# The second MLP of an attention and two-MLP kernel in six groups of 512 tokens in place of eight of 384

## The reference

```python
for t in range(S):                       # B, H, S, D = 4, 8, 768, 48
    cur = np.einsum('bhd,bhe->bhde', u[None] * kt, vt)
    y[:, :, t] = np.einsum('bhd,bhde->bhe', rt, state + cur)
    state = wt[:, :, :, None] * state + np.einsum('bhd,bhe->bhde', kt, vt)
x = attn_out.transpose(0, 2, 1, 3).reshape(B * S, H * D)      # (3072, 384)
h = x @ w_in;  g = where(h > 0, h, exp(min(h, 0)) - 1);  x = g @ w_out
h = x @ w_in2; g = h / (1 + exp(-1.702 * h));            out = g @ w_out2
```

## Time and profile before

| | |
|---|---|
| median of 3 runs | 1113.54 us (1112.53 to 1447.67) |
| span of the profiled execution | 1110.7 us |
| what lies around the span, by the median | 2.8 us |
| TensorE busy | 1047.1 us (94%) |
| VectorE busy | 645.4 us (58%) |
| ScalarE busy | 487.4 us (44%) |
| mean granted clock of TensorE | 0.972 |

### The profile page before, as it was taken

One profiled execution on the slowest core, in us unless ns is written; L12 is line 12 of the kernel. 1 busy time (PEld: TensorE's weight loads), 2 busy tenths in 40 slices (PEclk: granted clock), 3 DMA queues, 4 the chain that ended last, 5 costly groups with the idle time before them and its releaser, 6 DMA issues. The chain is left out here.

```text
span 1110.7 us, 27196 instructions
## 1 busy us (share of the span) xinstructions
PE 1047.1 (94%) x10912; PEld 946.3 (85%) x10912; DVE 645.4 (58%) x1587; ACT 487.4 (44%) x987; POOL 71.9 (6%) x55
## 2 busy tenths in 40 slices
PE   2658999999899999999999999999999999999998
PEld 1447878888788887778887799999999999999998
DVE  7997677677567677577676544343434433343433
ACT  2444455456245446346445357633333333333332
POOL 5450000000000000000000005410000000000000
PEclk9657999999999999999999999999999999999999
DMA  6453122212212212212211313300000000000000
GB/s 168 112 131 76 42 57 56 55 45 55 57 45 55 55 45 56 56 45 55 55 45 34 134 70 93 92 1 22 1 21 0 21 22 0 21 0 22 1 23 22
DMA packets 24096, 54.56 MB, mean 49 GB/s; under 512 B 3248, under 2 KB 15792, under 8 KB 23984
## 3 DMA queue, kind: packets, MB, share of 16 engines
q1 hardware_dynamic: 22704, 46.66, 16.1%
q0 software_dynamic: 1280, 6.29, 1.9%
HBM read 39.96 MB, written 12.98 MB: 48 GB/s over the span
## 5 line engine op out<-in xcount | busy, mean ns | idle before, releaser
L1200 PE MATMUL psum<-x_hi,w_split 128*128 128x384 f32 x912 | 232.6, 336 | 0.0
L1211 PE MATMUL psum<-g_hi,w_split 128*128 128x384 f32 x912 | 232.6, 336 | 0.0
L841 PE MATMUL psum<-g_hi,w_split 128*128 128x384 f32 x624 | 172.6, 348 | 0.0
L1200 PEld LDWEIGHTS psum<-x_hi,w_split 128*128 128x128 f32 x912 | 165.0, 188 | 0.0
L1211 PEld LDWEIGHTS psum<-g_hi,w_split 128*128 128x128 f32 x912 | 164.8, 188 | 0.0
L1118 DVE TENSOR_TENSOR gate<-expo,psum 128x384 f32<-128x384 f32 x128 | 70.9, 554 | 160.8 <-ACT expo L1037 160.8
L823 PE MATMUL psum<-x_hi,w_split 128*128 128x384 f32 x624 | 161.4, 340 | 0.0
L1200 PE MATMUL psum<-x_lo,w_split 128*128 128x384 f32 x456 | 153.6, 337 | 0.0
L1211 PE MATMUL psum<-g_lo,w_split 128*128 128x384 f32 x456 | 153.2, 336 | 0.0
L1037 ACT ACTIVATE expo<-psum 128x384 f32<-128x384 f32 x128 | 63.0, 492 | 170.6 <-PE psum L1200 170.6
L1124 DVE TENSOR_TENSOR g_lo<-gate,g_hi 128x384 fp32r<-128x384 f32 x152 | 84.9, 559 | 90.0 <-ACT g_hi L1044 90.0
(11 more groups left out here) (85 smaller groups left out, 1234.8 us busy)
## 6 DMA issues: line engine op xcount, KB each, us to landing
raw<-rkwu_dram SPq DMA_DIRECT2D x32, 288.4 KB, 5.5
staging<-weights_dram POOLq DMA_DIRECT2D x16, 384.0 KB, 3.7
raw<-rkwu_dram SPq DMA_DIRECT2D x32, 144.0 KB, 4.5
v_sb<-v_tokens_dram SPq DMA_DIRECT2D x16, 288.0 KB, 2.9
y_scratch<-y_sb SPq DMA_DIRECT2D x64, 72.0 KB, 1.8
staging<-y_scratch SPq DMA_DIRECT2D x7, 576.0 KB, 4.5
out_dram<-o_sb SPq DMA_DIRECT2D x7, 576.0 KB, 3.0
x_scratch<-x_sb SPq DMA_DIRECT2D x6, 576.0 KB, 3.4
```

The costliest lines, as they stand in the source:

```text
L841: mm = pe.matmul(mlp_bank(FT + m, x), w_tile((1 - x) * FT + f, lo, (KT + m) * P), gg[:, f, :], start=at == 0, stop=at == 3 * FT - 1)
L1200: mm = pe.matmul(hidden(f), w_tile(f, lo, kt * P), xx, start=n == 0, stop=n == 3 * KT - 1)
L1211: mm = pe.matmul(acc(q, m), w_tile(f, lo, (KT + m) * P), gg, start=f == first_tile(g) and n == 0, stop=f == NF - 1 and n == 2)
```

## The change

The second MLP has WIDES = 6 groups of WIDE = 512 tokens, so each of its matmuls has 512 columns, the width of a PSUM bank. `x2` becomes one row of tokens for each third of the features, from which a group takes 512 neighbours; three DMAs bring its six groups. `PAIRS` is 3. The first MLP keeps groups of 384.

To have the room, `gate2` has one buffer in place of two, and DVE waits for the low part of the tile before it writes the next gate; the two output buffers share their memory with `scores`, `kt_sb` and `state` of the attention; and `ur` (128 x 2 x 2 x 384) becomes `uk` (128 x 2 x 384): the bonus scales k, of which there is one array, and not r, which is laid out twice (once for each of two heads).

```diff
+WIDE = 512
+WIDES = B * S // WIDE
...
-        self.scores = sb("scores", [P, U, NG, CH])
-        self.kt_sb = sb("kt_sb", [P, U, NCH * P])
-        self.state = sb("state", [P, 2, U, NCH + 1, D])
+        pile = [sb(f"pile{q}", [P, KT * WIDE]) for q in range(2)]
+        self.scores = pile[0][:].rearrange("p (u g t) -> p u g t", u=U, g=NG)
+        self.kt_sb = pile[1][:, 0:U * NCH * P].rearrange("p (u n) -> p u n", u=U)
+        self.state = pile[1][:, U * NCH * P:].rearrange("p (x u c e) -> p x u c e", x=2, u=U, c=NCH + 1)
...
-    ur = sb("ur", [P, U, 2, HALF])
+    uk = sb("uk", [P, U, HALF])
...
-                act.activation(ur[:, u], r_of(x, u), ACT.Copy, scale=u_col(x, u)).then_inc(ur_done, 1)
+                act.activation(uk[:, u, :], k_of(x, u), ACT.Copy, scale=u_col(x, u)).then_inc(uk_done, 1)
...
-            dve.tensor_scalar(out=ur[:, 1], in0=r_of(0, 1), scalar1=u_col(0, 1), scalar2=None,
-                              op0=ALU.mult).then_inc(ur_done, 1)
+            dve.tensor_scalar(out=uk[:, 1, :], in0=k_of(0, 1), scalar1=u_col(0, 1), scalar2=None,
+                              op0=ALU.mult).then_inc(uk_done, 1)
...
-                                  kk[:, o:o + 32], ur[:, u, :, o:o + 32], start=True, stop=True)
+                                  uk[:, u, o:o + 32], r[:, :, o:o + 32], start=True, stop=True)
...
-    x2 = sb("x2", [P, GROUPS, KT * N])
-    expo = sb("expo2", [P, 2, N])
-    gate = sb("gate2", [P, 2, N])
-    g_hi = sb("g_hi2", [P, 4, N], F32R)
-    g_lo = sb("g_lo2", [P, 4, N], F32R)
-    o_sb = [sb(f"o_sb{q}", [P, KT, N]) for q in range(2)]
-    x_raw = o_sb[0]
+    x2 = sb("x2", [P, KT, GROUPS * N])
+    expo = sb("expo2", [P, 2, WIDE])
+    gate = sb("gate2", [P, WIDE])
+    g_hi = sb("g_hi2", [P, 4, WIDE], F32R)
+    g_lo = sb("g_lo2", [P, 4, WIDE], F32R)
+    o_sb = [z[:].rearrange("p (k n) -> p k n", k=KT) for z in kept.pile]
+    x_raw = kept.pile[0][:, 0:KT * N].rearrange("p (k n) -> p k n", k=KT)
...
-    hidden = lambda f: psum[:, f % 2, 0:N]
-    acc = lambda q, m: psum[:, 2 + 3 * q + m, 0:N]
-    PAIRS = GROUPS // 2
+    width = lambda second: WIDE if second else N
+    hidden = lambda f, second: psum[:, f % 2, 0:width(second)]
+    acc = lambda q, m, second: psum[:, 2 + 3 * q + m, 0:width(second)]
+    PAIRS = WIDES // 2
...
-            sp.dma_start(x2[:, 0:RIDERS, :], x2_dram.rearrange("g p n -> p g n")).then_inc(x2_in, 16)
+            for k in range(KT):
+                sp.dma_start(x2[:, k, 0:RIDERS * N].rearrange("p (g n) -> p g n", g=RIDERS),
+                             x2_dram[:, :, k * N:(k + 1) * N].rearrange("g p n -> p g n")).then_inc(x2_in, 16)
...
             def chain(g, f, second):
                 j = number(g, f)
+                if not (type(j) is int and j == 0):
+                    dve.wait_ge(lo_done, j)
                 dve.wait_ge(exp_done, j + 1)
                 if second:
-                    dve.tensor_tensor(gate[:, f % 2, :], expo[:, f % 2, :], hidden(f), ALU.mult).then_inc(gate_done, 1)
+                    dve.tensor_tensor(gate[:, 0:width(second)], expo[:, f % 2, 0:width(second)], hidden(f, second), ALU.mult).then_inc(gate_done, 1)
...
             with pe.Fori(0, PAIRS - 1) as b:
                 for q in range(2):
                     group(b * 2 + q + REST, q, True, True)
-            group(REST + GROUPS - 2, 0, True, True)
-            group(REST + GROUPS - 1, 1, True, None)
+            group(REST + WIDES - 2, 0, True, True)
+            group(REST + WIDES - 1, 1, True, None)
```

More of the change, by code:

```diff
@@ L734, in near @@
                 n = i * 2 + x
-                pe.wait_ge(ur_done, n * U + (U if first else u + 1))
+                pe.wait_ge(uk_done, n * U + (U if first else u + 1))
                 if not first:
                     pe.wait_ge(off_done, n * N_OFF - N_OFF + 2 * (u + 1))
-                kk = k_of(x, u)
+                r = r_of(x, u)
                 for c in range(NCH):
@@ L1036, in chain @@
                 if second:
-                    act.activation(expo[:, f % 2, :], hidden(f), ACT.Sigmoid, scale=1.702).then_inc(exp_done, 1)
+                    act.activation(expo[:, f % 2, 0:width(second)], hidden(f, second), ACT.Sigmoid, scale=1.702).then_inc(exp_done, 1)
                 else:
-                    act.activation(expo[:, f % 2, :], hidden(f), ACT.Relu, scale=-1.0).then_inc(neg_done, 1)
+                    act.activation(expo[:, f % 2, 0:width(second)], hidden(f, second), ACT.Relu, scale=-1.0).then_inc(neg_done, 1)
                     act.wait_ge(neg_done, j + 1)
-                    act.activation(expo[:, f % 2, :], expo[:, f % 2, :], ACT.Exp, scale=-1.0).then_inc(exp_done, 1)
+                    act.activation(expo[:, f % 2, 0:width(second)], expo[:, f % 2, 0:width(second)], ACT.Exp, scale=-1.0).then_inc(exp_done, 1)
                 act.wait_ge(gate_done, j + 1)
-                act.activation(g_hi[:, f % 4, :], gate[:, f % 2, :], ACT.Copy).then_inc(hi_done, 1)
+                act.activation(g_hi[:, f % 4, 0:width(second)], gate[:, 0:width(second)], ACT.Copy).then_inc(hi_done, 1)
             def evacuate(g, q, second, last=False):
@@ L1049, in evacuate @@
                     act.wait_ge(last_acc, 1)
-                    act.activation(o_sb[q][:, 0, :], acc(q, 0), ACT.Copy).then_inc(last_ready[0], 1)
+                    act.activation(o_sb[q][:, 0, :], acc(q, 0, second), ACT.Copy).then_inc(last_ready[0], 1)
                     return
@@ L1055, in evacuate @@
                 else:
-                    dst = x2[:, RIDERS + g, 0:N]
-                act.activation(dst, acc(q, 0), ACT.Copy).then_inc(out_ready if second else acc_act, 1)
+                    dst = x2[:, 0, (RIDERS + g) * N:(RIDERS + g + 1) * N]
+                act.activation(dst, acc(q, 0, second), ACT.Copy).then_inc(out_ready if second else acc_act, 1)
             def w2_high(f):
@@ L1197, in up, with down @@
                 for kt in range(KT):
-                    xh, xl = x_hi[q][:, kt * N:(kt + 1) * N], x_lo[q][:, kt * N:(kt + 1) * N]
+                    n0 = width(second)
+                    xh, xl = x_hi[q][:, kt * n0:(kt + 1) * n0], x_lo[q][:, kt * n0:(kt + 1) * n0]
                     for lo, xx in ((0, xl), (0, xh), (1, xh)):
-                        mm = pe.matmul(hidden(f), w_tile(f, lo, kt * P), xx, start=n == 0, stop=n == 3 * KT - 1)
+                        mm = pe.matmul(hidden(f, second), w_tile(f, lo, kt * P), xx, start=n == 0, stop=n == 3 * KT - 1)
                         n += 1
                 mm.then_inc(h_done, 1)
-            def down(g, q, f, last=False):
+            def down(g, q, f, second, last=False):
                 pe.wait_ge(lo_done, number(g, f + 1))
-                gh, gl = g_hi[:, f % 4, :], g_lo[:, f % 4, :]
+                gh, gl = g_hi[:, f % 4, 0:width(second)], g_lo[:, f % 4, 0:width(second)]
                 for m in range(KT):
                     for n, (lo, gg) in enumerate(((0, gl), (0, gh), (1, gh))):
-                        mm = pe.matmul(acc(q, m), w_tile(f, lo, (KT + m) * P), gg,
+                        mm = pe.matmul(acc(q, m, second), w_tile(f, lo, (KT + m) * P), gg,
                                        start=f == first_tile(g) and n == 0, stop=f == NF - 1 and n == 2)
@@ L1232, in group @@
                         up(g + 1, 1 - q, f + 2 - NF, False, following)
-                    down(g, q, f, last=following is None and f == NF - 1)
+                    down(g, q, f, second, last=following is None and f == NF - 1)
             for u in range(U):
@@ L1289 @@
             for n, a in arrays.items()]
[L1290 removed]
+    out = nc.dram_tensor("out_dram", (WIDES, DM, WIDE), F32, kind="ExternalOutput").ap()
     build(nc, *args, out)
```

60 lines of the change are left out of this document (32 added, 28 removed).

## The result

The changed kernel takes 1116.6 us (median of 12 runs, 1114.64 to 1117.63) against 1114.0 us for the kernel before beside it on the same chip: the ratio is 1.002, with a 95% interval of 1.001 to 1.0029. One of the 12 runs of before, at 1447.67 us, stands far off and is left out of the ratio. It is slower by 0.2%, where 0.7% faster was forecast, and 1116.6 us lies outside the range given (1098 to 1115).

What follows compares the result with a forecast made beforehand. The second MLP was taken as bound by TensorE's matmul stream. Terms of -7.7 (wide matmuls), -0.3 (bonus) and +0.3 us (tail) gave -7.7 us: 1103.0 + 2.8 = 1105.8 us, range 1098 to 1115.

Steps and rivals of the forecast that it cites:

- What bounds the kernel: Second MLP: a TensorE matmul stream at full clock, time being number times distance; 399.8 us, 36% of the span.
- Item 1: Second MLP on TensorE: 1728 wide matmuls at 226.9 ns, 392.1 us against 399.8, 7.7 us less.
- the readings: Extra of 13.6 ns per 384-column matmul: per matmul (chosen, 226.9 ns at 512), per column (231.5), or covered by wider matmuls.
- the stretch of 177 ns: From 655 to 695 us, 384-column matmuls came slower, at 177 ns; taken as sign of a price per matmul.
- (b): Second MLP: the extra is per column, 231.5 ns per wide matmul, nothing gained, 1113.5 us; chance 0.17.
- (c): Second MLP: wide matmuls cover the extra, 213.3 ns each, 31.2 us less, some 1082 us; chance 0.08.
- (d): Second MLP: the slow pattern stays, extra per matmul, 230.3 ns each, 398.0 us, total 1111.7 us; chance 0.08.
- (e): Second MLP: slow pattern with a price per column, 236 ns each, 8 us more, 1121.5 us; chance 0.05.
- Items 2, 3 and 4: Second MLP: longer ACT/DVE chain, one gate buffer, larger x splits and evacuations, all hidden behind TensorE; nothing counted.
- Item 5: Load of x2 by three DMAs with shorter pieces: transfer between 11.3 and 23.4 us, covered; nothing counted, 3 us at worst.
- Item 6: Attention part, bonus term on k: lighter preparations on ACT and DVE, 0.3 us less; ends 0 and 6.3.
- Item 7: Tail: a larger last copy on DVE and three stores of 256 KB in place of 192, 0.3 us more.

Runs made afterwards that it cites:

- m1: Matmuls alone, no kernel work, series of one width and type each: float32r 226.7 ns at 512 columns, 173.3 at 384; bfloat16 216.0 and 162.5.
- e6: Changed kernel with v_sb1 and wchunk1 allocated ahead of the weights, nothing added: 1105.4 us, 0.9923 of the kernel before.
- m2: TensorE series in the second MLP's order and nearly its addresses, no kernel work: 232.2 and 233.3 ns at 512 columns for the two x sets.
- e2: Changed kernel with each 512-column matmul of the second MLP as two of 256, each with its own load: 1125.8 us, 1.0108.
- e3: Changed kernel with the four ACT and DVE operations per tile of the second MLP on 64 of 512 columns: 1119.2 us, 1.0052.
- e1: Kernel before with only the bonus term moved to k, no wide groups: 1114.7 us against 1114.5, ratio 1.0002.
- m3: Matmuls alone with streaming row, weights or both shifted: at 512 columns 226.7 ns unshifted, 233.1 with row at 32 bytes, 226.8 with both.
- e4: Changed kernel with 32 unused bytes behind wchunk1, moving the second x set and gate parts against the weights: 1110.7 us, 0.9961.
- m4: Matmuls alone at more row-to-weight distances: at 512 columns 226.7 ns at 0 bytes, 233.3 at 32, 228.8 at 64, 227.1 at 256.

## Why the prediction was wrong, by its own steps

*What bounds the kernel* was right: the second MLP is a stream on TensorE at the full clock, without holes, before and after, and its time is number times distance.

*Item 1, 1728 x 226.9 ns,* is the step that failed: the term was mis-sized. It was to be 392.1 us and is 402.2: 10.1 us too little, more than the whole forecast gain of 7.7. The choice between the readings was right as far as it went. The extra that 384 columns have is a price per matmul of 13.3 ns (m1, at 256, 320, 384 and 512 columns; 16.0 at 448), a load of half the columns doesn't lower it, and e6, with the operands at a distance of 0, gives 226.7 ns and 1105.4 us where the sum had 226.9 and 1105.8. What was missing is a second extra that 384 columns don't have at the kernel's distance of 32 bytes and 512 do: 6.0 ns on average. No row of before could show it, since every matmul of both MLPs there has 384 columns.

*The argument from the stretch of 177 ns* reached the right reading by the wrong row. The prediction took it as a handover that had become dearer. m2 shows 384 columns locking into 173.3 or 176.7 ns by how a series starts, which says nothing about a price per column. The widths side by side (m1) decide it.

*The rivals.* The number of (b), 231.5 ns and 1113.5 us, came nearest, but its mechanism is false: m1 has 226.7 ns, and e2 is 9 us slower than after where it would have been level. (c), 213.3 ns and a little, is refuted by the 226.7 ns of m1. (d) had 230.3 ns from a pattern that lasts; a pattern that lasts is what the wide groups have, only its cause is the distance of the operands and not the stretch before them, as e3 shows: with 176.7 ns ahead of them the wide groups are the same as with 173.3. The deciding point of (e), 231.4 ns, was the right yardstick: 232.7 lies past it, hence slower.

*Items 2, 3 and 4,* the longer chain, the single gate buffer, the larger splits and evacuations at no cost: right. TensorE is busy 40.00 of 40 us, ACT and DVE wait 185 and 182 us for it, and a chain cut to an eighth (e3) changes no distance. Two figures of the working are slightly off and change nothing: ACT's work per tile adds up to 1.26 us, not 1.23, and DVE's 160.8 us over 121 times are 1.3 us each, not 1.4.

*Item 5,* the x2 in three DMAs at no cost: right. `up` waits 0.4 us for the last split, as before. The rows of the DMA issues (count, KB each, median us from issue to landing):
```profile
x<-x_scratch SPq DMA_DIRECT2D x3, 1152.0 KB, 8.3
```
That is the middle one; the last, issued at 628.9, landed 10.8 us later. So x2 was there 11.8 us after the first issue at 627.80, between the bounds (11.3 and 23.4 us) and close to the lower.

*Item 6,* 0.3 us less for the bonus on k: e1 has 1.0002 with an interval of 1.7 us to either side; a gain near the upper end of 6.3 us is excluded, 0.3 us can't be told from nothing. *Item 7:* 0.3 us more were forecast, 0.31 measured.

*The range* ended 1.5 us above rival (b), and (e), at 1121.5 us with a chance of 0.05, was left out of it. The result lies between the two. The readings were all made from one width, and the range took in only what they gave, nothing for an effect that first appears at the other width.

What stays open: why the distance costs what it does (the weights of the next matmul are loaded while the row streams, which m3 fits, but no run takes the load away), what the 13.3 ns are and why 448 and 496 columns have 16 to 17, and why set 0 in e4, with `up` at a distance of 0 and `down` at 64 bytes, has 230.4 ns (set 1, with both at 64, has the 228.9 that m4 leads one to expect). Whether all of the 2.2 us ahead of the MLPs is scatter isn't shown either.

## What to carry to other kernels

When an instruction gets a size that the trace doesn't have, run that size by itself and in the kernel's own places and order; a price fitted at one size is a guess at the other. When a stream of float32r matmuls of 512 columns has more than 226.7 ns from start to start, look at the distance between the weight tiles and the rows that stream, modulo 256 bytes: here a tensor of 24 bytes allocated between them cost 10.4 us, which is more than the wider matmuls gain, and moving it was free. A matmul that saves 13.3 ns by being one fewer needs many of its kind to pay, 576 here for 7.7 us; the type of the operands (bfloat16 has 10.7 ns less per matmul than float32r) was worth some 60 us here, 25 to 29 of them in the second MLP, where its coarser parts are allowed.

## What the runs showed that was not expected

- Float32r matmuls have 13.3 ns over columns / 2.4 GHz at four widths (16.0 at 448 columns), bfloat16 ones 2.5 to 2.7 ns. Half the weight columns don't lower the 13.3 ns; a row that repeats one element leaves 5.3 of them.
- With 512 columns of float32r the distance between weights and row matters, with a period of 256 bytes: 226.7 ns at 0, 228.8 at 64, 233.3 at 32, 238.2 at 4. With bfloat16 (216.0 ns at 32 bytes) it doesn't, with 384 columns hardly (173.3 to 175.5 ns), with 448 in part (206.4 ns at 32 bytes for 202.8).
- A stream can hold one of two rates with the same instructions: 384 columns at 173.3 or 176.7 ns, by how the series starts.
- With `down` at 32 bytes of distance, `up` beside it at 0 doesn't come back to 226.7 ns: the two in turn have 232.2 ns on average, `up` 231.0 and `down` 233.5. A change of distance also takes some matmuls to wear off: the last series of m4, at 0 behind one of 256 columns at 288, begins with eight distances of 228 to 236 ns before it holds 226.7, and `up` is only nine long. That this is the reason isn't shown.
